# Windowed attention and two MLPs on one core: one block sum earlier in six steps, two weight loads earlier in SP's queue, one copy earlier on ScalarE, a third warm-up matmul, and a buffer of constants padded to 512 bytes

## The reference

```python
scores = scale * np.matmul(q, k.transpose(0, 1, 3, 2)) + bias      # bias = -slope[h] * |i - j|
scores = np.where((rel >= 0) & (rel < 128), scores, -1e9)
attn = softmax(scores)
x = np.matmul(attn, v)                     # -> (2304, 512)
h = np.maximum(x @ w_in, 0.0);  x = h * h @ w_out        # first MLP
h = x @ w_in2;                  out = (h * np.cos(h)) @ w_out2   # second MLP
```

## Time and profile before

| | |
|---|---|
| median of three runs | 865.48 us (864.41 to 866.35) |
| the profiled execution's own time | 863.54 us |
| its span in the profile | 861.4 us |
| TensorE busy | 847.0 us (98%) |
| VectorE busy | 650.0 us (75%) |
| ScalarE busy | 525.9 us (61%) |
| GpSimd busy | 79.3 us (9%) |
| granted TensorE clock, mean | 0.998 |

### The profile page before, as it was taken

One profiled execution on the slowest core, in us unless ns is written; L12 is line 12 of the kernel. 1 busy time (PEld: TensorE's weight loads), 2 busy tenths in 40 slices (PEclk: granted clock), 3 DMA queues, 4 the chain that ended last, 5 costly groups with the idle time before them and its releaser, 6 DMA issues.

```text
span 861.4 us, 16166 instructions
## 1 busy us (share of the span) xinstructions
PE 847.0 (98%) x5844; PEld 766.3 (89%) x5844; DVE 650.0 (75%) x1455; ACT 525.9 (61%) x1145; POOL 79.3 (9%) x174
## 2 busy tenths in 40 slices
PE   6999999999999999999999999999999999999997
PEld 5888998999999999999999989899888898888896
DVE  6999978787687676696776777777877777767664
ACT  8999444342353333344333887777888877777774
POOL 7679500000000000000000000000000000000000
PEclk9999999999999999999999999999999999999999
DMA  7776725646588678678768555555565555665522
GB/s 241 229 245 185 271 97 194 229 163 244 211 293 303 247 281 312 248 247 317 282 239 296 185 194 177 168 195 196 193 224 195 190 177 183 219 231 165 193 74 74
DMA packets 72046, 185.34 MB, mean 215 GB/s; under 512 B 7200, under 2 KB 19488, under 8 KB 69920
## 3 DMA queue, kind: packets, MB, share of 16 engines
q1 hardware_dynamic: 71104, 183.23, 62.3%
q10 hardware_dynamic: 864, 1.08, 0.4%
HBM read 141.82 MB, written 42.47 MB: 214 GB/s over the span
## 4 chain that ended last, share of the span: by engine, by line
PE 91%; DVE 3%; ACT 2%; DMA 1%; issue 1%; POOL 0%; DVEq 0%
PE psum L692 39%; PE psum L726 22%; PE psum L731 15%; PE psum L733 8%; PE psum L630 4%; PE psum L588 3%; PE psum L533 2%; DMA wout_raw<-w_out 1%; DVE probs L1100 1%; DVE g_lo L1281 1%; DVE hidden_sum L1227 0%; PE psum L542 0%; ACT probs L820 0%; DMA k_raw<-k_t 0%; ACT xt_hi L881 0%
## 5 line engine op out<-in xcount | busy, mean ns | idle before, releaser
L692 PE MATMUL psum<-xt_hi,comb 128*128 128x384 f32 x1344 | 396.0, 337 | 2.5 <-DVE hidden_sum L1227 2.4
L692 PEld LDWEIGHTS psum<-xt_hi,comb 128*128 128x128 f32 x1344 | 247.4, 188 | 18.2 <-issue 4.1
L726 PE MATMUL psum<-wout,g_hi 128*128 128x512 f32 x576 | 180.2, 394 | 0.3 <-DVE g_lo L1281 0.3
L731 PE MATMUL psum<-g_hi,wout 128*128 128x512 f32 x384 | 149.8, 393 | 0.0
L921 ACT ACTIVATE g_hi<-work 128x384 fp32r<-128x384 f32 x192 | 97.2, 517 | 81.4 <-DVE work L1276 41.5
L1281 DVE TENSOR_TENSOR g_lo<-work,g_hi 128x384 fp32r<-128x384 f32 x192 | 102.4, 552 | 58.3 <-ACT g_hi L921 56.8
L692 PE MATMUL psum<-x_lo,comb 128*128 128x384 f32 x384 | 129.0, 336 | 0.0
L726 PEld LDWEIGHTS psum<-wout,g_hi 128*128 128x128 f32 x576 | 106.0, 188 | 12.7 <-issue 0.7
L726 PE MATMUL psum<-wout,g_lo 128*128 128x512 f32 x288 | 113.9, 396 | 0.0
L733 PE MATMUL psum<-g_hi,wout 128*128 128x256 f32 x384 | 107.9, 281 | 0.0
L692 PE MATMUL psum<-xt_lo,comb 128*128 128x384 f32 x288 | 96.8, 336 | 0.0
(11 more groups left out here) (94 smaller groups left out, 1279.6 us busy)
## 6 DMA issues: line engine op xcount, KB each, us to landing
comb<-comb SPq DMA_DIRECT2D x80, 768.0 KB, 4.9
wout<-wout SPq DMA_DIRECT2D x48, 512.0 KB, 4.9
comb<-comb SPq DMA_DIRECT2D x8, 1792.0 KB, 7.0
comb<-kept SPq DMA_DIRECT2D x8, 1792.0 KB, 6.8
wout_raw<-w_out SPq DMA_DIRECT2D x48, 256.0 KB, 6.0
comb<-comb SPq DMA_DIRECT2D x40, 256.0 KB, 3.1
v_raw<-v SPq DMA_DIRECT2D x16, 512.0 KB, 3.5
raw<-w_in SPq DMA_DIRECT2D x32, 256.0 KB, 7.1
```

Of the source, the lines that this page charges most:

```text
L692: last = pe.matmul(psum[:, H_BANK + i % 2, 0:NH], wi, mi[:, k, :], start=first, stop=True, skip_group_check=True)
L726: last = pe.matmul(psum[:, Y_BANK + c, :], g[:, r, tok], w, start=start and m == 0, stop=True, skip_group_check=True)
L731: pe.matmul(psum[:, Y_BANK + c, :], wi[:, w], g[:, r, 0:512], start=start and m == 0, stop=True, skip_group_check=True)
```

## The change

It has six parts. A third warm-up matmul is issued. The buffer of constants takes 512 bytes per partition instead of 32, so every buffer behind it moves by 480 bytes. On SP, `load_wout(5)` and `load_wout(4)` are issued in step 1 instead of step 2. On ScalarE, the first copy of the first pair's transposes stands behind two exponents of pair 2 instead of five. On VectorE, `c12_sum` of steps 1 and 2 stands ahead of two `lo_g`. And on VectorE, in the second step for each 768 tokens of the second MLP (steps 25, 33 and 41), `c21_sum` stands ahead of `make_g` and `c12_sum` ahead of `turn_high` and `turn_low` of the second block.

```diff
-WARM = 2
+WARM = 3
...
-        consts = place("consts", [P, 8], F32)
+        consts = place("consts", [P, P], F32)
...
-                if n >= 2:
+                if n == 1:
+                    load_wout(5)
+                    load_wout(4)
+                elif n > 2:
                     load_wout(2 * n + 1)
...
-                if n >= 2:
+                if n > 2:
                     load_wout(2 * n)
...
-                for u in ORDER[0:5]:
-                    exponent(s, u)
-                if s >= 2:
-                    copy_pt(s - 2, 0)
-                for u in ORDER[5:]:
+                for n, u in enumerate(ORDER):
+                    if s >= 2 and n == (2 if s == 2 else 5):
+                        copy_pt(s - 2, 0)
                     exponent(s, u)
...
                 make_g(n, 2)
+                if n <= 2:
+                    c12_sum(n)
                 lo_g(n, 0)
                 lo_g(n, 1)
-                c12_sum(n)
+                if n > 2:
+                    c12_sum(n)
                 make_g(n, 3)
...
                 if n < ALL:
+                    if j == 1:
+                        c21_sum(n)
                     make_g(n, 0)
-                    c21_sum(n)
+                    if j != 1:
+                        c21_sum(n)
                 if n > FRESH:
                     lo_g(n - 1, 3)
                 if n < ALL:
                     lo_g(n, 0)
+                    if j == 1:
+                        c12_sum(n)
                     turn_high(n, 1)
                     turn_low(n, 1)
-                    c12_sum(n)
+                    if j != 1:
+                        c12_sum(n)
                     turn_high(n, 2)
```

## The result

The changed kernel takes 858.38 us (median of 4, 857.85 to 858.65); the kernel before, with one more run, 865.47. The ratio is 0.992, 95% interval 0.9905 to 0.9936: 7.1 us faster, where 3.4 were forecast. The direction was right; the size is twice the forecast.

What follows compares the result with a forecast made beforehand. TensorE, busy 847.0 of 861.4 us, was taken as the bound, to be shortened where it stands still. Gains of 0.88 + 1.37 + 0.45 + 0.48 + 0.10 + 0.16 = 3.44 us gave 862.0, range 859.3 to 864.3.

Steps and rivals of the forecast that it cites:

- Step 2, 0.88: Start of step 2: with VectorE's c12 sum ahead of two g_lo rows, TensorE's whole hole of 0.88 us goes.
- Step 3, 1.37: Start of step 3: with the c12 sum moved up, 1.37 us gained of a 1.54 hole; a tenth stays.
- the gains are eaten: Rival: next limits stand close, at step 3 or inside steps 25, 33, 41; 863.2 or 864.3 us; chance 0.13.
- Steps 26, 34, 42: Starts of these steps: with the sum ahead of turn_high and turn_low, gains of 0.45, 0.48 and 0.10 us.
- SP's order: SP's queue, step 1: save of comb(2) and raw up to 3.7 us late, cover 1.8 or more; nothing taken.
- Attention, 0.16: Attention: 0.26 us gained by ScalarE's earlier copy in pair 2, less 0.1 for the third warm-up.
- The padding, nothing taken: Buffers behind consts move by 480 bytes; no cost or gain taken, as matmuls on moved and unmoved buffers looked equal.
- The bound of half a nanosecond: Resolution of the rows per matmul; on the two MLPs' 4,032 matmuls ±2.0 us, kept for the range.
- the gain 0.05: Rival on the buffers' places: new addresses save time per matmul, a gain of over 2 us more; chance 0.05.
- The base of the sum: Whole kernel: 3.44 us subtracted from the profiled execution, 863.54, giving 860.1, and from the median, 865.48, giving 862.0.
- brought forward by the third warm-up: Rival in attention: the third warm-up brings the faster clock forward, −0.5 us, 861.5; chance 0.12.

Runs made afterwards that it cites:

- filled wait: Kernel before plus four matmuls that nobody reads in TensorE's 2.2 us wait of pair 2: 863.40 us, ratio 0.9982.
- attention alone: Kernel before plus only the third warm-up and ScalarE's earlier copy in pair 2: 863.32 us, ratio 0.9983.
- the 3 single runs with the buffers apart: Changed kernel with the constants' buffer at 64, 544 or 384 bytes instead of 512: 864.15, 862.29 and 863.03 us.

## Why the prediction was wrong

Of the 7.1 us, 1.90 come from the closed holes at steps 2 and 3 and 1.07 from steps 26, 34 and 42 (VectorE's order alone). About 2.1 come from the places: from the start of step 0 to that of step 47 the changed kernel takes 2.11 less than the change without the padding, 0.053 for each step from 4 to 24 and 0.047 for nearly all later ones. Together that is the 5.1 by which the two profiled executions differ. The other 2.0 lie between before's profiled execution and its median, and I put them down to the fall of the clock in attention. That is in part argued. In the three later sets of runs before's executions with a fall took 1.5 to 2.3 us longer on average than those without; the clocks of the four runs behind 865.47 are not on record, but three of them took 865.4 or more, and in the later sets every execution of before above 864.6 had a fall. The gain of attention's own part isn't resolved.

Either of the two steps that failed below would alone have left the time within the range, the other terms as forecast: 862.0 less 2.1 is 859.9, less 2.0 is 860.0. Both together took it out.

Point by point:

- **Step 2, 0.88: right.** Step 1 became 0.81 shorter with VectorE's order alone, 0.86 in the changed kernel.
- **Step 3, 1.37: too large.** Steps 2 and 3 together gave 1.90 where 2.25 were forecast. I followed the sum that had been late and not the next row on VectorE that TensorE needs. The low part of comb ends at 122.32, hardly earlier than the 122.37 of before, and the new hole of 0.25, with the slow first matmul after it (0.1), is the missing 0.35. That was my rival "the gains are eaten" in a small form, but I had put it elsewhere. The hole itself is not the same in every execution: in the traces with before's order step 2 takes 15.08 us (filled wait), 15.50 (attention alone), 15.51 (before) and 15.91 (padding alone), as the second g_lo waits 0, 0.33, 0.35 and 0.77 for ScalarE's g_hi. With the sum moved up it takes 14.40 to 14.43 in all ten traces. So the forecast's remark that the move takes this wait out of TensorE's path was right, and a gain read from one trace of before is one draw.
- **Steps 26, 34, 42: right.** 0.44, 0.47, 0.16 against 0.45, 0.48, 0.10.
- **SP's order: right.** In the trace of the changed kernel SP's second wout load waits at the head and raw's second half goes out at 126.10 instead of 123.2, 2.9 later, against a bound of 3.7. VectorE starts on raw at 138.90 without a wait on it.
- **Attention, 0.16: not resolved.** The third warm-up cost 0.22 at the first scores (4.18 instead of 3.96), near the top of its bound. The scores then took 2.31 instead of 2.15 us; in other traces the same 32 take 2.00 (filled wait) and 2.63 (VectorE's order alone) with two warm-ups and 2.63 with three (attention alone), so this 0.16 can't be laid to the warm-up. The transposes that I had at 18.26 came at 18.64, later than before's 18.52, because ScalarE's copy itself moved to 18.02: the 0.38 by which this execution's first pairs ran later stood on every engine. Set against that, the copy did what was forecast: 18.52 and 0.38 are 18.90, and 18.64 is 0.26 earlier. The first hidden product came at 89.17 against 89.09. In other executions of changed versions without a fall it comes at 88.65 to 89.46, so a term of 0.16 can't be read; the 0.8 between the averages of the attention part alone and of before, without falls, isn't explained by it.
- **The padding, nothing taken: the first step that failed.** It is about 2.1 us. I compared the durations of two groups of matmuls, 335.9 and 336.1 ns, and concluded that both kinds of place cost the same. Two things were wrong with that. The matmuls overlap: a row's duration says little of how closely the next follows, and after the change the two means read 336 and 335 while the step is 53 ns shorter. And in the first MLP the rows that I compared, hidden products, are not where the time went. From start to start, over steps 5 to 21, the change without the padding and the changed kernel have 173.1 and 173.5 ns behind an xt_hi matmul, but 231.0 and 229.6 behind one of g_hi with 512 columns and 118.1 and 116.5 behind one with 256: the second products have all of it. The bound of half a nanosecond was close: 2.1 us over 4,032 matmuls is 0.52. I gave the gain 0.05 for want of a mechanism.
- **The base of the sum: the second step that failed.** I subtracted the same 3.44 from the profiled execution, 863.54, and from the median, 1.94 above it, and didn't ask what the 1.94 was. By the counts above it was the fall of the clock, absent from the one execution that I could see. In the executions without a fall the kernel before took 862.8 to 864.6, and the changed kernel 857.7 to 858.7. I had the clock only as "brought forward by the third warm-up", 0.5 at most. The run with two warm-ups shows that the third is not it, and the filled wait shows what is behind it: with TensorE kept at work there, the fall doesn't come. The Trainium skill says on "TensorE: Matmul & The Clock Gate", section "What's actually happening", that the throttled state is the default and that activity releases it. The filled wait agrees, 0 falls in 11 against 10 in 17.

Open: which part of the change keeps the clock up. With neither copy nor padding, 27 of before's 47 executions in the three later sets of runs fell and 3 of 5 with VectorE's order alone. With the copy, but not the padding, 3 of 11 (attention alone) and 3 of 6 (change without padding), and 2 of the 3 single runs with the buffers apart; with the padding alone, 4 of 10; with both, 1 of 15 (the changed kernel and its two warm-up version). That filling the wait keeps the clock up is shown. That copy and places together do it in the changed kernel is suggested by these counts and no more, and why of two executions with the same wait one falls and the other doesn't is not known. Open as well is which two streams collide when buffers don't start alike.

## What to carry to other kernels

When TensorE is 98% busy, its stream is the thing to measure: take the time between equal points of two equal steps far apart, not the duration of a row, and try the start of the buffers modulo 512 as a parameter of the kernel. Before a sum is set against a median, look whether the profiled execution belongs to the median; where executions of one kernel fall into two groups, find out which one the profile is. And when a wait is removed, follow the waiting engine to its next input on the same queue: here it was a few rows further down.

## What the runs showed of the hardware

Buffers that start alike modulo 512 bytes made a step of the first MLP 15.600 us, buffers 32 bytes apart 15.653, 64 apart 15.732, 384 apart 15.737. The Trainium skill gives the gap between isolated matmuls ("TensorE: Matmul & The Clock Gate", section "Back-to-back issue gap") by a formula in the number of columns, with no address in it. Here the spacing also went by where the operands lie, by up to 0.9% of a step.

The granted clock fell to its lower level of 1.2 GHz near 17 us of the span, and rose again after 20 us, in more than half of the executions of the kernel before by the count above; in the trace of VectorE's order alone the fall came right after a wait of 2.2 us. Four matmuls without a reader in that wait took the fall away at no cost that the trace shows, and left a spread of 1.2 us (862.67 to 863.85) where before has 3.7 (862.77 to 866.49).
